# Splitting the state product of a gated linear attention over four quarters of TensorE's array

## The reference

```python
state = np.zeros((B, H, D, D), dtype=np.float32)      # B, H, S, D = 4, 8, 768, 48
for t in range(S):
    state = alpha[:, :, t, :, None] * state + np.einsum('bhd,bhe->bhde', k[:, :, t], v[:, :, t])
    y[:, :, t] = np.einsum('bhd,bhde->bhe', q[:, :, t], state)
x = np.ascontiguousarray(attn_out.transpose(0, 2, 1, 3)).reshape(B * S, H * D)   # 3072 x 384
h = x @ w_in;  r = np.maximum(h, 0.0);  x = (r * r) @ w_out      # 384 -> 2048 -> 384
h = x @ w2_in; g = h * (1.0 / (1.0 + np.exp(-h))); out = g @ w2_out
```

## Time and profile before

| | |
|---|---|
| median of 3 runs | 915.03 us (914.72 to 915.25) |
| the profiled execution, own time | 913.71 us |
| its span (first to last instruction) | 912.1 us |
| TensorE busy | 891.1 us (98%) |
| VectorE, ScalarE, GpSimd busy | 435.6, 403.6, 75.8 us |
| granted TensorE clock | full in all 40 slices |

### The profile page before, as it was taken

How to read it: one execution, slowest core, us unless ns; L and a number is a source line. 1 busy time by engine, 2 the same in 40 slices (tenths; PEclk the granted TensorE clock), 3 DMA queues, 4 the chain that set the end, 5 groups by cost and what they waited for, 6 DMA issues and landing times.

```text
span 912.1 us, 12930 instructions
## 1 busy us (share of the span) xinstructions
PE 891.1 (98%) x4882; PEld 742.6 (81%) x4882; DVE 435.6 (48%) x658; ACT 403.6 (44%) x754; POOL 75.8 (8%) x107
## 2 busy tenths in 40 slices
PE   6799999999999999999999999999999999999997
PEld 5587878888888888888888888888888888888897
DVE  7788996687778677664343311312212212212310
ACT  4675554445445444544666632333323323233520
POOL 3564300000000000001123000000000000000000
PEclk9999999999999999999999999999999999999999
DMA  9596343224232432301232300200200201100100
GB/s 168 156 258 141 86 115 86 64 64 112 67 79 67 115 74 64 98 18 51 70 123 89 102 1 1 64 7 1 70 1 13 57 1 36 35 1 0 35 10 29
DMA packets 103571, 59.90 MB, mean 66 GB/s; under 512 B 55600, under 2 KB 95152, under 8 KB 103504
## 3 DMA queue, kind: packets, MB, share of 16 engines
q1 hardware_dynamic: 97056, 51.25, 23.3%
q0 software_dynamic: 2048, 6.29, 2.2%
q10 hardware_dynamic: 4400, 1.48, 0.9%
HBM read 45.02 MB, written 9.44 MB: 60 GB/s over the span
## 4 chain that ended last, share of the span: by engine, by line
PE 95%; SPq 3%; DMA 1%; issue 1%; ACT 0%; DVE 0%; DVEq 0%; ACTq 0%
PE h_ps L733 43%; PE z_ps L747 40%; PE job_ps L765 3%; PE job_ps L664 2%; PE job_ps L717 2%; SPq L357 2%; PE job_ps L713 2%; PE job_ps L675 1%; PE z_ps L765 1%; PE job_ps L686 1%; DMA x_raw<-y_sb 1%; SPq L394 0%; SPq L346 0%; DVE qp L1105 0%; ACT x_hi L997 0%
## 5 line engine op out<-in xcount | busy, mean ns | idle before, releaser
L1191 DVE TENSOR_TENSOR g_lo<-g,g_hi 128x512 fp32r<-128x512 f32 x177 | 121.5, 687 | 357.4 <-ACT g_hi L948 243.0
L733 PE MATMUL h_ps<-x_hi,win_hi 128*128 128x512 f32 x576 | 224.8, 390 | 2.6 <-DVE x_lo L1183 1.8
L733 PE MATMUL h_ps<-x_lo,win_hi 128*128 128x512 f32 x576 | 224.1, 389 | 0.0
L733 PE MATMUL h_ps<-x_hi,win_lo 128*128 128x512 f32 x576 | 224.1, 389 | 0.0
L943 ACT ACTIVATE g<-h_ps 128x512 f32<-128x512 f32 x96 | 57.4, 598 | 232.1 <-PE h_ps L733 232.1
L945 ACT ACTIVATE g<-h_ps 128x512 f32<-128x512 f32 x96 | 57.3, 597 | 183.8 <-PE h_ps L733 161.0
L733 PEld LDWEIGHTS h_ps<-x_hi,win_hi 128*128 128x128 f32 x576 | 108.1, 188 | 25.9 <-DVE x_lo L1183 2.3
L733 PEld LDWEIGHTS h_ps<-x_hi,win_lo 128*128 128x128 f32 x576 | 108.1, 188 | 22.5
L733 PEld LDWEIGHTS h_ps<-x_lo,win_hi 128*128 128x128 f32 x576 | 108.1, 188 | 22.3
L747 PE MATMUL z_ps<-g_hi,wout_hi 128*128 128x512 f32 x288 | 116.4, 404 | 0.0
L948 ACT ACTIVATE g_hi<-g 128x512 fp32r<-128x512 f32 x177 | 111.8, 632 | 5.6
(11 more groups left out here) (135 smaller groups left out, 864.3 us busy)
## 6 DMA issues: line engine op xcount, KB each, us to landing
z_scratch<-z_sb SPq DMA_DIRECT2D x18, 256.0 KB, 2.7
x_raw<-z_scratch SPq DMA_DIRECT2D x6, 768.0 KB, 4.5
v_sb<-in_v SPq DMA_DIRECT2D x44, 96.0 KB, 2.5
out_x<-z_sb SPq DMA_DIRECT2D x80, 48.0 KB, 1.7
nat_a<-in_alpha SPq DMA_DIRECT2D x40, 88.0 KB, 2.2
nat_k<-in_k SPq DMA_DIRECT2D x40, 88.0 KB, 2.2
nat_q<-in_q SPq DMA_DIRECT2D x40, 88.0 KB, 2.3
x_raw<-y_sb SPq DMA_DIRECT2D x34, 96.0 KB, 2.3
```

The costliest lines, as they stand in the source:

```text
L733: last = nc.tensor.matmul(h_ps[f % 2][:], w[:, f, tile(kk)], x[par][:, kk, :], start=(kk == TILES[0] and n == 0), stop=(kk == TILES[-1] an ...
L1191: nc.vector.tensor_tensor(low, g[f % 2][:], high.bitcast(F32), ALU.subtract).then_inc(g_lo_made, 1)
```

## The change

For pairs 4 to 23 the product of the state is cut into 8 products of 48 rows: one for each head and batch. The head chooses the row half of the array, and the batches go two and two to the column halves (batches 0 and 1 to partitions 0 to 63, batches 2 and 3 to 64 to 127), so that each product fills one quarter. The two heads write two banks, `job_ps[2]` and `job_ps[0]`. The values' products follow the same layout: head by bank, batch half by column half. ScalarE copies two halves of 256 columns in place of 512 columns at once, and every piece that moves to `x_raw` is two DMAs of half the columns.

```diff
-        def y_bank(n):
-            return z_ps[1] if n < PAIRS else job_ps[2]
+        first_y, later_y = z_ps[1], (job_ps[2], job_ps[0])
...
+            def repack_halves(p):
+                for row, kk, to, n in repack_pieces(p):
+                    h, r = divmod(row, 64)
+                    for i, cols in enumerate((slice(0, UT // 2), slice(UT // 2, UT))):
+                        sp.dma_start(x_raw[to:to + n, kk, cols], y_sb[p % 2][64 * i + r:64 * i + r + n, h * UT // 2:(h + 1) * UT // 2]
+                                     ).then_inc(y_moved[p % 2], 16)
...
                     wait(sp, y_copied, y_count(n + 1))
-                    repack(n % PAIRS)
+                    repack_halves(n % PAIRS)
...
-                    for b in range(BATCH):
-                        nc.tensor.matmul(ps[0:ROWS, tile(b)], state[:, p, b, :], qp[n % 2][:, tile(b)],
-                                         start=(b == 0), stop=False, skip_group_check=True)
...
+            def y_halves(n):
+                p = n % PAIRS
+                if n < 2 * PAIRS:
+                    wait(pe, first_made, 2 * (n - PAIRS + 1))
+                wait(pe, state_made, 2 * (n - 2 * PAIRS + 1))
+                if has_state(n):
+                    wait(pe, kt_copied, n + 1)
+                v_flat = v_tile(n).rearrange("t b h d -> t (b h d)")
+                places = [(half, h, 2 * half + odd, 64 - 16 * half) for odd in (0, 1) for half in (0, 1) for h in (0, 1)]
+                def to(half, h, b, cols):
+                    return later_y[h][64 * half:64 * half + cols, tile(b % 2)]
+                for half, h, b, cols in places:
+                    at = (p * BATCH + b) * ROWS + 64 * h
+                    nc.tensor.matmul(to(half, h, b, cols), flat_state[head_rows(h), at:at + cols], qp[n % 2][head_rows(h), tile(b)],
+                                     start=(b % 2 == 0), stop=False, skip_group_check=True)
+                for odd in (0, 1):
+                    for h in (0, 1):
+                        for half, b, cols in ((0, odd, 64), (1, 2 + odd, HD)):
+                            at = (2 * b + h) * HD
+                            last = nc.tensor.matmul(to(half, h, b, cols), v_flat[:, at:at + cols], score[h][:, b, :],
+                                                    start=False, stop=True, skip_group_check=True)
+                last.then_inc(y_made, 1)
...
-                nc.scalar.activation(y_sb[n % 2][:], y_bank(n)[0:ROWS, :], ACT.Copy).then_inc(y_copied, 1)
+                half = UT // 2
+                nc.scalar.activation(y_sb[n % 2][:, 0:half], later_y[0][0:ROWS, 0:half], ACT.Copy)
+                nc.scalar.activation(y_sb[n % 2][:, half:UT], later_y[1][0:ROWS, 0:half], ACT.Copy).then_inc(y_copied, 1)
```

More of the change, by code:

```diff
@@ L120, in moved @@
     per_pair = [len(repack_pieces(p)) for p in range(PAIRS)] + [0] * 2
+    unmoved = per_pair[PAIRS - 1] if pair % 2 else 0
+    whole, part = sum(per_pair[pair % 2::2]), sum(per_pair[pair % 2:pair:2])
     if is_first(units):
[L122 to L125, removed]
+        return 16 * part
+    if isinstance(units, int) and units <= UNITS:
+        return 16 * (2 * whole * (units - 1) + whole - unmoved + 2 * part)
+    return 16 * (whole * (units - UNITS) + 2 * whole * (UNITS - 1) + whole - unmoved + part)
 def wait(eng, sem, value):
@@ L693, in y_stage @@
                 wait(pe, masked, 2 * (n + 1))
[L694 to L698, removed]
+                if n >= PAIRS:
+                    y_halves(n)
+                    if has_state(n):
+                        i_stage(n)
+                    return
+                ps = first_y
+                wait(pe, y_copied, n)
+                wait(pe, scanned, 2 * BATCH)
                 if n == PAIRS - 1:
@@ L717, in y_stage @@
                         last = nc.tensor.matmul(ps[head_rows(h), tile(b)], v_tile(n)[:, b, h, :], score[h][:, b, :],
-                                                start=(n < PAIRS and b == 0), stop=True, skip_group_check=True)
+                                                start=(b == 0), stop=True, skip_group_check=True)
                 last.then_inc(y_made, 1)
-                if n >= PAIRS and has_state(n):
-                    i_stage(n)
+            def y_halves(n):
[3 more added lines that the diff above has]
+                wait(pe, state_made, 2 * (n - 2 * PAIRS + 1))
+                if has_state(n):
+                    wait(pe, kt_copied, n + 1)
[14 more added lines that the diff above has]
+                last.then_inc(y_made, 1)
             def stage(kind, n):
@@ L798, in _ @@
                     pe.wait_ge(held_made, 2)
+                    pe.wait_ge(y_copied, y_count(LASTP + 1))
                     nc.tensor.matmul(job_ps[0][0:1, 0:1], all_held[:], ones[:], start=True, stop=True).then_inc(held_summed, 1)
@@ L898, in y_copy @@
                 wait(act, y_made, n + 1)
-                nc.scalar.activation(y_sb[n % 2][:], y_bank(n)[0:ROWS, :], ACT.Copy).then_inc(y_copied, 1)
+                if n < PAIRS:
+                    nc.scalar.activation(y_sb[n % 2][:], first_y[0:ROWS, :], ACT.Copy).then_inc(y_copied, 1)
+                    return
+                half = UT // 2
+                nc.scalar.activation(y_sb[n % 2][:, 0:half], later_y[0][0:ROWS, 0:half], ACT.Copy)
+                nc.scalar.activation(y_sb[n % 2][:, half:UT], later_y[1][0:ROWS, 0:half], ACT.Copy).then_inc(y_copied, 1)
             def split_w(n, hi, turned, arrived):
@@ L998, in _ @@
             act.wait_ge(y_made, PAIRS)
-            nc.scalar.activation(x_hi[0][0:EDGE, 0, :], y_bank(PAIRS - 1)[0:EDGE, :], ACT.Copy).then_inc(x_hi_made, 1)
+            nc.scalar.activation(x_hi[0][0:EDGE, 0, :], first_y[0:EDGE, :], ACT.Copy).then_inc(x_hi_made, 1)
             kt_copy(PAIRS - 1)
@@ L1213, in _ @@
             dve.wait_ge(x_hi_made, KD)
-            nc.vector.tensor_tensor(x_lo[0][0:EDGE, 0, :], y_bank(PAIRS - 1)[0:EDGE, :], x_hi[0][0:EDGE, 0, :].bitcast(F32),
+            nc.vector.tensor_tensor(x_lo[0][0:EDGE, 0, :], first_y[0:EDGE, :], x_hi[0][0:EDGE, 0, :].bitcast(F32),
                                     ALU.subtract).then_inc(x_lo_made, 1)
```

## The result

The changed kernel takes 910.18 us (median of 5 runs, 909.07 to 911.67), the kernel before 914.72 us (5 runs, 912.61 to 915.25). The ratio is 0.9955, with a 95% interval of 0.9935 to 0.9974: 4.5 us less by the medians, 4.1 by the ratio, where 4.8 were forecast.

What follows compares the result with a forecast made beforehand. TensorE, 98% busy, was taken as the bound. State's products and way in fall from 0.97 to 0.68 us; with 0.01 for weights each stage saves 0.28, 17 count: 915.03 - 4.8 = 910.2 us, range 907.6 to 913.6.

Steps and rivals of the forecast that it cites:

- Four quarters at a time: State's products in stage Y: 16 quarter records, four at a time, take four rounds of 0.109 us, 0.436 in all.
- The run: State's products in stage Y: 0.436 us of rounds, 0.10 for leaving and 0.05 for the start.
- the way in: Stage Y, from the last hidden-block product to the state's products: 0.32 us against 0.23, so 0.09 more, as at S.
- a full drain: Last 512-column product must end before the quarters start: way in 0.39 us, stage 0.21 shorter, total 911.5; the trace suggested cheaper.
- Loads are hidden: State's products: the rival, each round showing a 0.05 us load, gives 913.6 us; chance 0.08 with other in-between paces.
- 17 of 20 stages: Savings at Y of pairs 4, 7, 8 only lengthen waits at S of pairs 5, 9; 17 x 0.28 = 4.8 us.
- the saving of a period: Each four-step period from pair 9 on gets 0.28 us shorter, fitting into VectorE's 0.61 us of room.
- the slow side: Outcomes slower than before, chance 0.12 in one place; the range leaves out the slow side with 0.13.
- its rivals: Two quarters at a time (917.6 us, chance 0.11); loads shown (913.6, 0.08); VectorE or moves take more back (911.5 to 913, 0.05).
- The rest of the change: ScalarE's halved copies and 50 more DMAs on SyncE's queue: covered by waits, so they cost nothing.
- The wait for the moves: ScalarE at the end of the first unit: its 1.68 us wait grows by 1.2 us from two more issues.
- cover: End of the first unit: x_lo's first third done at 116.6, VectorE comes at 118.09, so 1.5 us are left.

## Why the prediction was right

- **Four quarters at a time.** The run was summed as 0.436 + 0.10 + 0.05 = 0.59 and took 0.59; the way in was summed as 0.32 and took 0.32. That the rounds are what counts is shown from both sides: two quarters with the same records, and four quarters with twice the records, both take 1.02 us.
- **The way in has the price that S showed.** The quarters start 0.32 us behind the last product, as S did, and not at its recorded end, 0.39 behind its start. The Trainium skill says that changing the tiling mode drains TensorE ("TensorEngine Tiling (Array Packing)", Key Properties), and gives no price. The price here is 0.09 us between two starts. The prediction called this cheaper than a full drain; since the profile models the ends of products, the 0.39 isn't measured, and whether the 0.09 is itself a drain stays open.
- **Loads are hidden.** The Trainium skill says that loads overlap matmuls in flight only where the row group differs ("TensorE: Matmul & The Clock Gate", Part 3, The mechanism). This case doesn't agree: two quarters share their rows, and a round takes 0.11 us; with a load of 0.05 shown in each, it would be 0.16.
- **17 of 20 stages.** Shown by place: the same added work costs 0.1 us in the trace at pairs 4, 7 and 8 and 2.6 us at pairs 10 to 12; moving S of pair 9 gave the savings of pairs 7 and 8 back. That pairs 9 to 19 have little room left is shown by the kernel without the state's products, which waits at every S from pair 10 to pair 20. And with the products made twice, which adds 0.43 us to every stage, the trace is 7.3 us longer than the changed kernel's, 17 times 0.43.
- **The size.** The forecast was 4.8 us and the medians give 4.5. The term that was a little off is the saving of a period, taken as 0.28: from pair 9 on it is 20.55 (174.75 - 154.20 in the trace of before) less 20.29, that is 0.26. The stage alone did get 0.28 shorter (58.30 to 60.40 is 2.10, 59.57 to 61.39 is 1.82, to the start of L686 and L695); 0.02 come back elsewhere in the period, and where was not found out. The last three periods, which have no increment of the state, are 0.31 shorter. The whole adds up: 13 periods at about 0.26, three at 0.31 and some 0.3 for the last stage Y are 4.6, and the 0.13 by which the two stretches with the long waits grew leaves 4.5. (In the prediction's last sum the slow side has a chance of 0.12 and then of 0.13; its rivals add up to 0.13.)
- **The rest of the change costs nothing that can be measured.** By itself it gives a ratio of 0.9991, not to be told from 1, as forecast. The wait for the moves was mis-sized, at 1.2 us more where 0.60 were measured (0.85 in the kernel with the moves alone), so that 1.8 us of cover were left where 1.5 were reckoned. The copy in two halves ended 0.66 us after its start (111.84 to 112.50), 0.06 later than in one.
- **The hundredth of agreement is partly luck.** The forecast of 910.2 us was made from a median of 3 runs, and the measured 910.18 is a median of 5 that spread over 2.6 us, against a kernel before that came out at 914.72 and not at 915.03. What agrees within the noise is the difference, 4.5 us for 4.8.

## What to carry to other kernels

Price a split of the array in rounds: the longest list of records on one tile, times the time of one record, plus some 0.25 us for going in, starting and leaving (0.11 us a record and 0.25 us are what these float32 products of 128 columns took); a short run of small products gains only as far as the rounds saved are worth more than that. Then ask for each instance which wait comes next: a saving that lies between two points which another engine's unbroken chain ties together is worth nothing, and the cure is work placed ahead of the wait, if that engine has idle time behind it; if not, the delay comes back at the next wait, as at pair 6. A saving per period has a ceiling as well: read the distance from the last release to the start that it permits, here 0.61 us before and 0.36 after, and take off the 0.10 that remains even where TensorE waits. Compare two profiles by distances inside the part that changed, since the clock ahead of it can differ between executions.

## What the runs showed of the hardware

- **A quarter did not wait for the order of the program.** With all eight records of one column half ahead of the other half's, both halves ran together, in 0.59 us as with the alternating order, and four of the first eight records to start were of the second half.
- **The clock falls in some executions and not in others.** In two of the profiled executions the granted clock fell for a time just behind a wait at S. These are the stretches of the kernel with the other order of quarters (wait of 1.75 us at S of pair 9, at 133.57), the row of the S that follows, and the stretch of the kernel without the state's products (S of pair 5):

```profile
130.00:150.00 20.00, 18.25 (x126) 14.70 (x125) 12.89 (x19) 9.28 (x19) 0.00 (x0) 0.91 0.34 97
...
133.57 1.16 PE L673 MATMUL job_ps<-qp,kp 48*128 48x128 f32 x16 [1.75 <-issue]
155.49 1.16 PE L673 MATMUL job_ps<-qp,kp 48*128 48x128 f32 x16
```

```profile
60.00:76.00 16.00, 13.98 (x94) 11.51 (x94) 14.71 (x22) 10.05 (x22) 8.06 (x6) 0.91 1.03 246
```

  The columns ahead of the last two are busy times, and 0.91 is the mean granted clock: a part of the stretch at 1.2 GHz in place of 2.4. From S of pair 9 to S of pair 10 it is 21.92 us there against 20.29 in the changed kernel, 1.6 us lost. The changed kernel's own profile, with the same wait of 1.74, shows no fall there. But it shows the one at 42 us, ahead of S of pair 4, a short time after TensorE had waited 1.66 us for GpSimd's part of `x_lo`; the profile of before has a wait of 1.85 us in that region and no fall. So it is a matter of the execution, and that waits cause it was not tried. It goes with the spread of the runs, in both kernels: of the five runs of the changed kernel the one with a mean clock of 1.000 took 909.07 us and the one with 0.996 took 911.67, and of 18 runs of the kernel before the three with 0.995 took 916.62 to 917.32, the one with 1.000 took 913.22.
